# Attention and two feed-forward layers: the second half of the attention pipeline runs one step later, and the queue of loads is reordered

## What is computed

```python
scores = scale * np.matmul(q, k.transpose(0, 1, 3, 2))
cum = np.cumsum(np.maximum(s, 0.0), axis=-1)
scores = np.where(causal, -1e9, scores + np.minimum(-(cum[..., :, None] - cum[..., None, :]), 0.0))
attn = exp(scores - max); attn = attn / (sum + 1e-09)
x = np.matmul(attn, v)            # heads put side by side: 2304 x 512
xn = x / sqrt(mean(x * x) + 1e-06) * rms_g
x = (silu(xn @ w_gate) * (xn @ w_val)) @ w_out        # d_ff 1536
h = x @ w_in;  out = (h - tanh(h)) @ w_out2           # d_ff 2048
```

## Time and profile before

| | |
|---|---|
| median of three executions | 1107.17 us |
| profiled execution | 1106.37 us |
| its span | 1104.6 us |
| TensorE busy | 1065.3 us, 96% |
| VectorE, ScalarE, GpSimd busy | 39%, 38%, 16% |
| starts of the scores of pairs 1 to 6 (k) | 22.82, 35.16, 49.09, 62.77, 78.41, 92.84 us |
| starts of pairs 9, 10 | 134.64, 147.16 us |
| starts of pairs 13, 14, 15 | 188.04, 203.68, 220.53 us |
| TensorE's first feed-forward product | 234.88 us |
| last product with V | 244.0 us |

### The profile page before, as it was taken

The page is one execution under the profiler, slowest core; times in us unless marked ns, Lnnn a source line. Parts: engine busy times, 40 slices in busy tenths (PEclk is TensorE's granted clock), DMA queues, the critical chain, the costliest instruction groups (busy, mean ns, idle before and its releaser), DMA issues.

```text
span 1104.6 us, 18165 instructions
## 1 busy us (share of the span) xinstructions
PE 1065.3 (96%) x6516; PEld 980.2 (89%) x6516; DVE 431.2 (39%) x1203; ACT 421.1 (38%) x1030; POOL 172.2 (16%) x184
## 2 busy tenths in 40 slices
PE   5888998899999999999999999999999999999998
PEld 4767777689999999999999999999999999999997
DVE  6656666654432222322322333533223232332322
ACT  5666677663431232222222233533223232322322
POOL 8767777640000000000000000000000000000000
PEclk9999999999999999999999999999999999999999
DMA  6555555322200000000000122210000000000000
GB/s 198 171 167 171 172 172 172 112 75 82 65 1 1 1 0 0 0 0 0 0 0 0 29 77 86 87 30 29 1 1 29 0 28 0 0 28 0 28 0 28
DMA packets 61251, 56.40 MB, mean 51 GB/s; under 512 B 7598, under 2 KB 51630, under 8 KB 61194
## 3 DMA queue, kind: packets, MB, share of 16 engines
q1 hardware_dynamic: 61194, 55.67, 16.5%
HBM read 41.63 MB, written 4.87 MB: 42 GB/s over the span
## 4 chain that ended last, share of the span: by engine, by line
PE 91%; DMA 2%; issue 2%; DVE 2%; POOL 1%; ACT 1%; SPq 0%; DVEq 0%; ACTq 0%; POOLq 0%
PE HP L958 15%; PE HP L960 15%; PE HP L959 15%; PE YP L959 11%; PE YP L960 11%; PE YP L958 11%; PE OP L927 5%; PE TP L911 4%; PE SC L896 3%; PE SC L897 2%; DMA RB<-PT 1%; DMA Qraw<-in_qT 1%; POOL KD L399 1%; DVE PR L675 1%; DVE PT L698 0%
## 5 line engine op out<-in xcount | busy, mean ns | idle before, releaser
L958 PE MATMUL HP<-XS,WA 128*128 128x384 f32 x576 | 194.6, 338 | 0.0
L960 PE MATMUL HP<-XS,WA 128*128 128x384 f32 x576 | 193.0, 335 | 0.0
L959 PE MATMUL HP<-XS,WA 128*128 128x384 f32 x576 | 192.7, 335 | 0.0
L777 DVE TENSOR_TENSOR AC<-AC,HP 128x384 f32<-128x384 f32 (+2 forms) x78 | 40.3, 522 | 293.4 <-PE HP L960 293.4
L828 DVE TENSOR_TENSOR AC<-HP,AC 128x384 f32<-128x384 f32 (+1 forms) x108 | 54.3, 512 | 216.3 <-ACT AC L603 216.3
L603 ACT ACTIVATE AC<-HP 128x384 f32<-128x384 f32 x96 | 47.2, 492 | 215.9 <-PE HP L960 215.4
L958 PEld LDWEIGHTS HP<-XS,WA 128*128 128x128 f32 x576 | 108.2, 188 | 2.6 <-issue 0.2
L959 PEld LDWEIGHTS HP<-XS,WA 128*128 128x128 f32 x576 | 108.2, 188 | 2.4
L911 PE MATMUL TP<-ident,PR 128*128 128x128 f32 (+1 forms) x480 | 86.8, 285 | 23.3 <-issue 16.6
L960 PEld LDWEIGHTS HP<-XS,WA 128*128 128x128 f32 x576 | 108.1, 188 | 0.0
L541 ACT ACTIVATE AC<-HP 128x384 f32<-128x384 f32 x72 | 35.4, 492 | 177.8 <-PE HP L960 177.8
(11 more groups left out here) (105 smaller groups left out, 1979.4 us busy)
## 6 DMA issues: line engine op xcount, KB each, us to landing
X<-in_w SPq DMA_DIRECT2D x52, 256.0 KB, 3.0
Kraw<-in_kT SPq DMA_DIRECT2D x16, 576.0 KB, 4.7
Qraw<-in_qT SPq DMA_DIRECT2D x16, 576.0 KB, 5.7
out_rows<-OS SPq DMA_DIRECT2D x18, 256.0 KB, 2.2
QO<-QA SPq DMA_DIRECT2D x15, 288.0 KB, 3.4
Vt<-in_v SPq DMA_DIRECT2D x16, 256.0 KB, 3.0
WRAW<-in_w SPq DMA_DIRECT2D x16, 256.0 KB, 4.3
RB<-PT SPq DMA_DIRECT2D x128, 32.0 KB, 2.2
```

What stands on the lines that cost most here:

```text
L777: dve.tensor_tensor(AC[:, m % 2, cols], AC[:, m % 2, cols], HP[:, 1, cols], ALU.mult).then_inc(prod_done if part is None else prod_part, 1)
L958: pe.matmul(dst, w(0), x(0), start=start, stop=False)
L959: pe.matmul(dst, w(0), x(1), start=False, stop=False)
L960: return pe.matmul(dst, w(1), x(0), start=False, stop=stop)
```

## The change

Transposes, copies, products with V and output multiplications each run one step later behind the scores: the lags are 3, 4 and 5. PR gets a fourth buffer, indexed by n % 4. The mean square of the last batch moves from step 8 to step 9. VectorE's output multiplication is put at the end of its step, behind both minima and both copies. In SyncE's list K and Q of the pair after next are issued at the head of the pair (u = 0), behind KD and ahead of all RB loads of the pair; QO goes ahead of the RB load in u = 1; V moves from u = 3 to u = 4. The hand-over to the feed-forward layers has one step more to drain and is interleaved with `gate(0, 0)` and `value(0, 0)` in another order.

```diff
--- before.py
+++ after.py
@@ -33,11 +33,11 @@
 SLOT = 2 * DM
 M_ATT = B * PAIRS // 2
 
-T_LAG, V_LAG, O_LAG = 2, 3, 4
+T_LAG, V_LAG, O_LAG = 3, 4, 5
 RBS = 3
 ALL = B * STEPS
 
-SQ_STEPS, MS_STEP, ROOT_STEP = (0, 1, 2, QB), 8, 2 * QB
+SQ_STEPS, MS_STEP, ROOT_STEP = (0, 1, 2, QB), 9, 2 * QB
 RINV = 4
 
 SPLITS1 = [(0, 1), (2, 3), (4, 5), (6, 7), (8, 9), (10, 11), (12, 13), (14, 15), (16, 17), (18, 19), (), ()]
@@ -145,7 +145,7 @@
         KA = sb("KA", [P, 2, 2, S], F32R)
         KD = sb("KD", [P, 2, 2, S], F32R)
         Vt = sb("Vt", [P, 2, QB, 2 * D], F32)
-        PR = sb("PR", [P, 3, 2, PAD + S], F32)
+        PR = sb("PR", [P, 4, 2, PAD + S], F32)
         PT = sb("PT", [P, 3, 2, QB * P], F32)
         NM = sb("NM", [P, 4, 2], F32)
         RS = sb("RS", [P, 4, 2, 2], F32)
@@ -315,11 +315,6 @@
                 if u == 0 and k + 1 < B * PAIRS:
                     wait(sp, scores_done, 2 * QB * k)
                     load_decay(*at)
-                if n >= T_LAG:
-                    load_rb(n - T_LAG)
-                if u == 1 and k + 1 < B * PAIRS:
-                    sp.wait_ge(q_hi, 2 * (k + 2))
-                    load_qo(*at)
                     if k + 2 < B * PAIRS:
                         if k == 0:
                             sp.wait_ge(qo_first, 2)
@@ -329,12 +324,17 @@
                             sp.wait_ge(k_lo, 2 * k)
                             sp.wait_ge(q_lo, 2 * k)
                         load_qk(*after, k % 2)
-                if u == 3 and k + 1 < B * PAIRS:
-                    wait(sp, pv_done, QB * k)
-                    load_v(*at, (k + 1) % 2)
+                if u == 1 and k + 1 < B * PAIRS:
+                    sp.wait_ge(q_hi, 2 * (k + 2))
+                    load_qo(*at)
+                if n >= T_LAG:
+                    load_rb(n - T_LAG)
                 if u == 2 and 0 < k < B * PAIRS - 1:
                     sp.wait_ge(w_lo, k)
                     load_weights(*at)
+                if u == 4 and k + 1 < B * PAIRS:
+                    wait(sp, pv_done, QB * k)
+                    load_v(*at, (k + 1) % 2)
             for n in range(ALL - T_LAG, ALL):
                 load_rb(n)
 
@@ -456,7 +456,7 @@
             def exponential(b, n, hh):
 
                 _, z, nk, _ = q_block(n % QB)
-                pr = PR[0:z, (b * STEPS + n) % 3, hh, PAD:PAD + nk]
+                pr = PR[0:z, n % 4, hh, PAD:PAD + nk]
                 act.wait_ge(mins_done, b * 2 * STEPS + 2 * n + hh + 1)
                 act.activation(pr, pr, ACT.Exp, bias=NM[0:z, n % 4, hh:hh + 1], scale=-1.0,
                                accum_out=RS[0:z, n % 4, hh, 0:1]).then_inc(exp_done, 1)
@@ -479,7 +479,7 @@
 
                 z = q_block(n % QB)[1]
                 act.wait_ge(recip_done, b * STEPS + n + 1)
-                act.activation(PR[0:z, (b * STEPS + n) % 3, :, 0:PAD], RR[0:z, n % 4].rearrange("p (h o) -> p h o", o=1).broadcast_to([z, 2, PAD]), ACT.Copy
+                act.activation(PR[0:z, n % 4, :, 0:PAD], RR[0:z, n % 4].rearrange("p (h o) -> p h o", o=1).broadcast_to([z, 2, PAD]), ACT.Copy
                                ).then_inc(pad_done, 1)
 
             def square(c, t):
@@ -667,12 +667,12 @@
                 u = n % QB
                 _, z, nk, _ = q_block(u)
                 dve.wait_ge(scores_done, b * 2 * STEPS + 2 * n + hh + 1)
-                wait(dve, t_done, b * NG + groups_of(n - 3, 1)[-1][0] + 1)
+                wait(dve, t_done, b * NG + groups_of(n - 4, 1)[-1][0] + 1)
                 dve.nop(nofuse=True)
                 bank, halves = score_bank(u, hh), nk // (nk if nk <= BANK else nk // 2)
                 sc = SC[0:z, bank:bank + halves, 0:nk // halves]
                 end = S - P + z
-                dve.tensor_tensor_reduce(PR[0:z, (b * STEPS + n) % 3, hh, PAD:PAD + nk].rearrange("p (a f) -> p a f", a=halves), sc,
+                dve.tensor_tensor_reduce(PR[0:z, n % 4, hh, PAD:PAD + nk].rearrange("p (a f) -> p a f", a=halves), sc,
                                          mask[0:z, end - nk:end].rearrange("p (a f) -> p a f", a=halves),
                                          -SCALE, 3.0e38, ALU.add, ALU.min, accum_out=NM[0:z, n % 4, hh:hh + 1]
                                          ).then_inc(mins_done, 1)
@@ -734,16 +734,15 @@
                     p, u = n // QB, n % QB
                     for hh in range(2):
                         minima(b, n, hh)
-                        if hh == 0:
-                            if n >= 1 or not first:
-                                recip(b, n - 1)
-                            if n >= O_LAG or not first:
-                                output(b, n - O_LAG)
+                        if hh == 0 and (n >= 1 or not first):
+                            recip(b, n - 1)
                         if n >= T_LAG or not first:
                             evacuate(b, n - T_LAG, hh)
                         if last and n == MS_STEP and hh == 0:
                             dve.wait_ge(ms_done, 1)
                             dve.tensor_copy(SQ[:, 0], MS).then_inc(ms_read, 1)
+                    if n >= O_LAG or not first:
+                        output(b, n - O_LAG)
                     if last:
                         for t in range(1, KT):
                             if n == SQ_STEPS[t] + 1:
@@ -909,7 +908,7 @@
                         if j == 0:
                             pe.wait_ge(pad_done, b * STEPS + n + 1)
                         last = pe.transpose(TP[:, g % 2, i * P:i * P + z],
-                                            PR[0:z, (b * STEPS + n) % 3, hh, j * P:(j + 1) * P], ident[0:z, 0:z])
+                                            PR[0:z, n % 4, hh, j * P:(j + 1) * P], ident[0:z, 0:z])
                     last.then_inc(t_done, 1)
 
             def values(b, n):
@@ -979,14 +978,17 @@
 
 
             for hh in range(2):
-                transposes(B, -2, hh)
+                transposes(B, -3, hh)
+            values(B, -4)
             pe.wait_ge(mins_done, 2 * B * STEPS)
             pe.wait_ge(w_lo, B * PAIRS)
             gate(0, 0)
+            for hh in range(2):
+                transposes(B, -2, hh)
             values(B, -3)
+            value(0, 0)
             for hh in range(2):
                 transposes(B, -1, hh)
-            value(0, 0)
             values(B, -2)
             values(B, -1)
```

## The result

| | before | after |
|---|---|---|
| median of runs, us | 1107.24 (1105.19 to 1108.59, 4 runs) | 1148.68 (1143.04 to 1152.12, 4 runs) |
| profiled execution, us | 1106.37 | 1143.04 |
| its span, us; mean granted clock | 1104.6; 0.997 | 1141.3; 0.976 |

What follows compares the result with a forecast made beforehand. Bound: TensorE's work, about 12 us a pair, plus one wait for RB behind K and Q. From 1106.4, minus 9.2 (pairs 1 to 12), 1.4 (pair 13), 2.2 (pair 14), plus 0.4 (end): 1094.0, as median 1095 us; range 1086 to 1108.

Steps and rivals of the forecast that it cites:

- the new wait: TensorE before products x20 in step 3, waiting for block 2's output multiplication: 0.45 to 0.5 us a pair.
- K's issue: SyncE's queue: K goes out 3.3 us after the pair's start, behind V and KD.
- TensorE's arrival at the products x20: Step 3 of a pair: TensorE gets there 9.25 us after the pair's start.
- The wait at the pair's head: TensorE waits for VectorE's copy before the first transposes x3: 0.4 us a pair, between 0 and 1.0.
- Pair 14: Pair with the root: about 1 us less idle time and 1.2 us less slow clock, 2.2 us gained.
- when the RB loads of block 2 have landed: End of step 2: 6.0 us after K's issue, so RB is usable at 9.3 us in the pair.
- The upper bound: Time from K's issue to RB: at most 7.37 us, the worst of before, with 6.76 as the ordinary one.
- The slower rival: RB of block 2 at 7.37 us: TensorE's step 3 wait grows to 1.9 us, 1113 us in all; chance 0.14.
- the slow clock: TensorE's lower clock after a 2.2 us idle adds 1.2 us to a pair; less likely with 0.5 us waits.
- the prediction's own chain: A pair: 12.0 us of work plus waits of 0.5 and 0.5 us, 13.0 us against 13.77.
- W = 12.0: TensorE's work in a pair, taken as 12.0 us, between 11.8 and 12.26.
- the end: Hand-over after the last transposes: a loss of 0.4 us, between 0 and 1.5.

Runs made afterwards that it cites:

- the first experiment: The changed kernel with SyncE's loads in the order of the kernel before, lags and VectorE's order as changed: 1093.3 us, ratio 0.986 to before.

## Why the prediction was wrong

**What held.** That the feed-forward layers give nothing; that TensorE's idle time hangs on the RB behind K and Q; the place of the new wait, K's issue (3.14 us against 3.3) and TensorE's arrival at the products x20 (9.32 against 9.25). The wait at the pair's head was forecast as 0.4: it is 0.40 to 0.44 in four of the pairs 1 to 12 and 0.2 or less in the others, but 0.43 to 0.46 in nearly every pair of the first experiment, where no other wait covers it. Pair 14 gains 1.9 us against 2.2, but in another way: idle time falls by 0.3 us (forecast 1.0) and busy time, at a granted clock of 1.00 in place of 0.90, by 1.6 (forecast 1.2). That this number fits is in part luck.

**The step that failed: when the RB loads of block 2 have landed.** The prediction took 6.0 us from K's issue, between 5.44 and 7.37; measured are 7.94 to 9.83, with 8.46 in the median. TensorE's wait ahead of the products x20, forecast as 0.5 us, became 2.1 to 4.0 in nine of the pairs 1 to 12. Three mistakes made this size:

- It took QO's new place as a gain and V's as harmless ("issued 1.8 us before K"). The runs show both as costs: V's 288 KB, in rows of 512 bytes just ahead of K, cost 1.1 us (V back in step 3), and QO, behind Q and two RB loads, 0.4 to 0.5 (QO in step 2, with and without V ahead).
- The upper bound was not the highest of the trace before. It holds a longer case, 7.62 us, and the median of its pairs with such a wait is 6.85 and not 6.76. Its timelines of SyncE and VectorE:

```profile
167.33 0.53 SPq L262 DMA_DIRECT2D Kraw<-in_kT  x1
```
```profile
174.95 0.23 DVE L713 TENSOR_TENSOR X<-OP,RB 128x64 f32<-128x64 f32 x1 [0.55 <-DMA RB<-PT]
```

- The bounds came from another queue order than the new one, and still the range was closed at them. The slower rival named this mechanism and its place, and "V in small rows directly ahead of K", but stopped at 7.37 us. It also named the slow clock and left it out of its sum: 1.2 us in each of twelve pairs is 14 us that its 1113 does not hold.

K landed 4.7 us after its issue in both kernels; the whole difference comes behind it, with Q, which took 5.7 us before and takes 7.4 now. What happens in between can only be made out in part, from the DMA rows of the two kernels, 9 us each from 0.8 us before K's issue on, in 40 slices (busy tenths of the 16 engines, GB/s). Before:

```profile
DMA  0000009979595999989999999999988447899521
GB/s 0 7 2 0 0 0 328 205 143 225 102 246 143 369 389 430 430 328 389 369 328 492 369 389 369 336 280 436 396 289 248 153 125 225 255 241 278 169 77 43
```

After:

```profile
DMA  0040397996799969879997998879997627534394
GB/s 0 5 121 21 96 278 218 316 372 233 266 369 410 307 246 328 287 287 389 328 369 287 314 266 269 360 287 246 194 178 132 150 75 205 139 96 107 71 178 157
```

Before, the engines are idle when K is issued and then full until K and Q are through, some 5.8 us after the issue. After, V's larger part, issued 1.1 us ahead of K, lands 1.8 us behind K's issue, and for the last 2.7 us the rate is 70 to 210 GB/s, in most of the last 2 us with 60% of the engines busy or less. This looks as if K and Q were through on some engines and not on others, but the rows do not show the engines singly. The Trainium skill (DMA: Bandwidth & Descriptors, section Queues, rings and completion order) says that a DMA is split over up to 16 rings, that each engine consumes its own in order, and that the semaphore's part of an engine comes after its earlier writes; the half-empty slices agree with that. By that rule an RB load is complete only when its slowest part is. Which ring is behind, why V makes them uneven, and whether it is V's small rows or its bytes that do it, no run here shows.

**The clock came on top.** With waits of 2.1 to 4.0 us ahead of the products x20 in nine of the twelve pairs, most pairs hold a stretch at the lower level (1.2 GHz): busy time is 13.77 in the pair shown and 14.08 in the mean of pairs 2 to 12, where 12.21 is enough at 1.00. With 8.46 in place of 6.0 the prediction's own chain gives a wait of 3.3 + 8.46 + 0.4 - 9.25 = 2.9 us, and with its price of the slow clock a pair of 12.0 + 0.5 + 2.9 + 1.2 = 16.6; measured are 16.62 in the mean. So the chain of steps was right and one term carried the sign: even without the slow clock that sum is 15.4, slower than the 13.77 of before. That the sum fits so closely is luck in part: the wait is 2.2 us a pair in the mean (26.7 / 12) and the clock costs up to 1.9.

**Two smaller slips.** W = 12.0 rests on transposes that are "drawn out" after a wait, 0.63 us against 0.49. The two numbers come from two views, the timeline and the chain; in the timeline x4 takes as long without a wait:

```profile
105.98 0.66 PE L911 MATMUL TP<-ident,PR 128*128 128x128 f32 x4
```

TensorE is busy for 12.21 us in an undisturbed pair with the new lags. And the end costs 2.4 us, where the forecast was 0.4 and at most 1.5; it costs 2.2 in the first experiment as well and nothing with VectorE's order alone, so it goes with the lags and not with SyncE's order.

**What was not seen.** The prediction priced VectorE's order at 0.2 us in a pair. It is the only part that gains: 21 us alone, 14 on top of the lags, 12 on top of SyncE's new order. The earlier trace rows show it: VectorE's wait of 1.73 us has a minimum and a copy behind it, TensorE's 1.86 us follow. The prediction read these rows so itself, and then priced the move by the 0.2 us of the multiplication, not by the wait ahead of it. The cure was to take the copy out from behind the waiting instruction, not to move RB.

## What to carry to other kernels

A small load that is soon wanted must not stand behind large ones, and what a large load costs depends on what is just ahead of and behind it in the queue; a bound taken from the old order of a queue is none for a new one, so leave the range open on that side. Put an instruction that may wait at the end of its engine's step, behind the work that others wait for: here two moved lines gave 1.9%, and the deeper pipeline beside them nothing. Look for every instruction that waits for a load, also by the slot that the load reads. Try such parts alone, since one part's loss (55 us) hid the gain of the rest (16 us).

## What the runs showed of the hardware

Loads of 576 KB are slowed by their neighbours in one queue, by amounts that add: 1.1 us for 288 KB in 512-byte rows issued 1.1 to 1.7 us ahead, 0.4 to 0.5 for 288 KB from SBUF to SBUF some 2 us behind (K to RB; by the landing of Q 1.1 to 1.2 and 0.6 to 0.7). TensorE's granted clock stayed at 1.00 in pairs of the kernel before with single waits of up to 1.86 us and was 0.89 in the one with 2.17. It was 0.78 to 0.90 in the mean of the changed kernel's pairs 2 to 12, most of which hold a wait of 2 us and more; the lowest, 0.78, belongs to a pair without such a wait that follows one with 2.26. A pair's order of work alone changed its length by 0.5 us (12.29 against 12.76), of which only 0.15 shows as idle time of TensorE.
